# Attention outputs of the first token tile kept on chip, their stores moved to another queue, and five weight splits moved

## The reference

```python
def _attn_ref(q, k, v):                       # q, k, v: 8 x 8 heads x 576 x 64, float32
    scores = scale * np.matmul(q, k.transpose(0, 1, 3, 2))
    Dmat = np.where(rel >= 0, gamma[:, None, None] ** rel[None, :, :], 0.0)
    return np.matmul(scores * Dmat[None, :, :, :], v)
def _moe_ref(x, w1, w2, w3, w_out):           # x: 4608 x 512, d_ff 768
    h = np.maximum(np.maximum(x @ w1, x @ w2), x @ w3)
    return h @ w_out
def _moe2_ref(x, w1, w2, w3, w_out):          # d_ff 1024
    a = x @ w1
    b = x @ w2
    h = a * b @ w3
    return h @ w_out
```

## Time and profile before

| | us |
|---|---|
| median of 3 runs | 1257.79 |
| lowest, highest run | 1256.33, 1263.64 |
| profiled execution | 1263.11 |
| its span, first to last instruction | 1261.3 |
| first matmul of stage B starts at | 193.04 |

### The profile page before, as it was taken

How to read it: one execution, slowest core, us unless ns; L and a number is a source line. 1 busy time by engine, 2 the same in 40 slices (tenths; PEclk the granted TensorE clock), 3 DMA queues, 4 the chain that set the end, 5 groups by cost and what they waited for, 6 DMA issues and landing times. The chain is left out here.

```text
span 1261.3 us, 21125 instructions
## 1 busy us (share of the span) xinstructions
PE 1229.0 (97%) x8288; PEld 1211.0 (96%) x8288; DVE 774.1 (61%) x1186; ACT 487.2 (39%) x771; POOL 434.0 (34%) x228
## 2 busy tenths in 40 slices
PE   7899999999999999999999999999999999999999
PEld 7798889999999999999999999999999999999998
DVE  5565676764645454558789767554545465867563
ACT  3333344432323242426455444242424243545441
POOL 2635536502020202033786564202020216266540
PEclk9899999999999999999999999999999999999999
DMA  9899865212020302033545441212121343444441
GB/s 328 313 333 349 297 235 160 86 47 79 26 101 26 100 26 95 32 126 126 192 163 198 163 169 57 102 64 106 50 101 57 107 156 123 151 150 151 156 157 64
DMA packets 87828, 174.15 MB, mean 138 GB/s; under 512 B 9648, under 2 KB 58416, under 8 KB 87728
## 3 DMA queue, kind: packets, MB, share of 16 engines
q1 hardware_dynamic: 79088, 163.94, 37.0%
q10 hardware_dynamic: 8640, 8.85, 2.0%
HBM read 109.32 MB, written 63.44 MB: 137 GB/s over the span
## 5 line engine op out<-in xcount | busy, mean ns | idle before, releaser
L1057 PE MATMUL ps<-chi,whi 128*128 128x384 f32 x2016 | 675.5, 335 | 11.6 <-DVE clo L795 5.9
L1059 PE MATMUL ps<-chi,wlo 128*128 128x384 f32 x2016 | 674.1, 334 | 0.0
L1058 PE MATMUL ps<-clo,whi 128*128 128x384 f32 x2016 | 674.1, 334 | 0.0
L554 POOL TENSOR_TENSOR raw<-raw,raw 128x768 f32<-128x768 f32 (+2 forms) x96 | 267.3, 2804 | 591.5 <-DMA raw<-xd 222.1
L1057 PEld LDWEIGHTS ps<-chi,whi 128*128 128x128 f32 x2016 | 378.9, 188 | 15.8 <-issue 7.9
L1058 PEld LDWEIGHTS ps<-clo,whi 128*128 128x128 f32 x2016 | 378.9, 188 | 0.0
L1059 PEld LDWEIGHTS ps<-chi,wlo 128*128 128x128 f32 x2016 | 378.9, 188 | 0.0
L795 DVE TENSOR_TENSOR clo<-raw,chi 128x768 fp32r<-128x768 f32 (+2 forms) x168 | 251.9, 1527 | 27.7 <-ACT chi L712 27.7
L712 ACT CAST chi<-raw 128x768 fp32r<-128x768 f32 (+2 forms) x168 | 180.3, 1080 | 86.0 <-PE ps L1059 52.3
L785 ACT COPY w<-ps 128x384 f32<-128x384 f32 x126 | 60.7, 482 | 253.4 <-PE ps L1059 252.0
L771 ACT COPY u<-ps 128x384 f32<-128x384 f32 x126 | 60.8, 482 | 161.8 <-PE ps L1059 160.1
(11 more groups left out here) (41 smaller groups left out, 857.0 us busy)
## 6 DMA issues: line engine op xcount, KB each, us to landing
qks<-qk SPq DMA_DIRECT2D x32, 576.0 KB, 7.0
gd<-h SPq DMA_DIRECT2D x96, 192.0 KB, 1.9
raw<-gd SPq DMA_DIRECT2D x24, 768.0 KB, 5.9
hd<-h SPq DMA_DIRECT2D x72, 192.0 KB, 1.9
raw<-hd SPq DMA_DIRECT2D x24, 576.0 KB, 5.6
vs<-vv SPq DMA_DIRECT2D x32, 320.0 KB, 8.4
raw<-xd SPq DMA_DIRECT2D x24, 384.0 KB, 5.7
x2d<-h SPq DMA_DIRECT2D x48, 192.0 KB, 2.1
```

Of the source, the lines that this page charges most:

```text
L554: return nc.gpsimd.tensor_tensor(out_, a, b, op)
L1057: nc.tensor.matmul(to, w1, x1, start=(start and k == 0), stop=False, skip_group_check=True)
L1058: nc.tensor.matmul(to, w1, x2, start=False, stop=False, skip_group_check=True)
L1059: last = nc.tensor.matmul(to, w2, x1, start=False, stop=(k == KH[st] - 1), skip_group_check=True)
```

## The change

1. **The first tile stays on chip.** `TILE0` lists, for batches 0 and 1, which columns of a pair belong to tile 0. `read_values` copies them from PSUM into the blocks `raw[B]` themselves, in place of `xst`. Pairs 0 to 3 are wholly in tile 0 (two copies, of 384 and 192 columns, no store). Of pairs 4 to 7, 192 columns are (one copy there, one of 384 columns into `xst`, one store). `load_raw(0)` is gone; what waited for it waits for the copies.
2. **Stores from SP, three buffers.** `xst` has three buffers and all 52 stores are issued by SP, in the step's order behind the `vs` load of the same turn. `ks` moves behind u3, uo and the weights.
3. **Values without zero rows.** `vs` is loaded as 128 rows of 512 (`vv`) and 64 rows of 128 (`vt`); DVE zeroes the rest once (six memsets).
4. **Splits moved.** Weights 9, 10, 19 and 20 are split one iteration earlier, 11, 12 and 13 at another place (both halves at the end of `it` where they were in `it` and `it`+1); weight 20 is loaded one iteration earlier; three entries of stage O's table of token splits are moved (`HI_IO`, `LO_IO`).

```diff
-HI_IO = {("prev", "w"): [0], ("end", "u"): [1], ("end", "p3"): [2], ("end", "p2"): [3],
+HI_IO = {("prev", "p3"): [0], ("end", "u"): [1], ("end", "p3"): [2], ("end", "p2"): [3],
...
-LO_IO = {("end", "21"): [0], ("end", "12"): [1], ("next", "22"): [2, 3], ("next", "12"): [4, 5, 6]}
+LO_IO = {("prev", "12"): [0], ("end", "12"): [1], ("next", "22"): [2, 3], ("next", "21"): [4],
+         ("next", "12"): [5, 6]}
...
-             18: 69, 19: 109, 20: 112}
+             18: 69, 19: 109, 20: 111}
...
-W_SPLIT_AT = {wi: it + (wi >= FIRST_W[C]) for wi, it in W_SUM_AT.items()}
+W_SPLIT_AT = {wi: it + (FIRST_W[I] <= wi < FIRST_W[O]) for wi, it in W_SUM_AT.items()}
+
+AT_ONCE = (11, 12, 13)
...
-P1_RAW = 9
+
+TILE0 = [[(0, N, {0: 0, 1: 2}, 0), (N, SEQ, {0: 3, 1: 6}, 0)], [(0, 2 * N - SEQ, {0: 3, 1: 6}, SEQ - N)]]
+X_STORES = [0 if n < PAIRS else 1 if n < 2 * PAIRS else 2 for n in range(NP)]
...
-        xst = at("xst", [P, 2, SEQ], f32, H_AT)
+        xst = at("xst", [P, 3, SEQ], f32, A21_AT + 3 * KH[B] * P * 4)
...
-                sp.dma_start(vs[n % 6][:, :], vv[n, :, :]).then_inc(v_loaded[n % 6], 16)
+                sp.dma_start(vs[n % 6][:, 0:NC * CH], vv[n, :, :]).then_inc(v_loaded[n % 6], 16)
+                sp.dma_start(vs[n % 6][TAIL:P, NC * CH:], vt[n, :, :]).then_inc(v_loaded[n % 6], 16)
...
             for m in range(STEPS):
-                for n in made_in(m + 1):
-                    load_k(n)
                 if m in U3_LOAD:
                     load_u3(U3_LOAD[m])
...
                 if m in P1_W_LOAD:
                     load_weight(P1_W_LOAD[m])
-                if m == P1_RAW:
-                    load_raw(0)
+                for n in made_in(m + 1):
+                    load_k(n)
                 for n in made_in(m + 2):
                     load_qk(n)
                 for n in (2 * m, 2 * m + 1):
                     if n + 4 < NP:
                         load_v(n + 4)
+                    if n - 2 >= PAIRS:
+                        store_x(n - 2)
...
             def read_values(n):
+                b, p = divmod(n, PAIRS)
                 act.wait_ge(valued, n + 1)
-                if n >= 2:
-                    act.wait_ge(x_stored[n % 2], 32 * (n // 2))
-                nc.scalar.copy(xst[:, n % 2, :],
-                               ps[:, 2 * (n % 2):2 * (n % 2) + 2, :].rearrange("p a b -> p (a b)")[:, 0:SEQ]
-                               ).then_inc(x_out, 1)
...
+                x = ps[:, 2 * (n % 2):2 * (n % 2) + 2, :].rearrange("p a b -> p (a b)")
+                in_tile = TILE0[b] if b < 2 else []
+                for i, (lo, hi, block, to) in enumerate(in_tile):
+                    copy = nc.scalar.copy(raw[B][block[p // 2]][:, p % 2, to:to + hi - lo], x[:, lo:hi])
+                if X_STORES[n]:
+                    if n - 3 >= PAIRS:
+                        act.wait_ge(x_stored[n % 3], 16 * x_stores(n - 3))
+                    lo = in_tile[-1][1] if in_tile else 0
+                    copy = nc.scalar.copy(xst[:, n % 3, lo:SEQ], x[:, lo:SEQ])
+                copy.then_inc(x_out, 1)
...
                 for wi in range(2, NW):
-                    if W_SPLIT_AT.get(wi) == it - 1:
+                    if W_SPLIT_AT.get(wi) == it - 1 and wi not in AT_ONCE:
                         split_weight(wi, 0)
...
+                for wi in AT_ONCE:
+                    if W_SPLIT_AT[wi] == it:
+                        split_weight(wi, 0)
+                        split_weight(wi, 1)
```

More of the change, by code:

```diff
@@ L189, with x_stores @@
 P1_W_LO = {12: (0, 0), 13: (0, 1), 14: (1, 0), 15: (1, 1)}
-P1_RAW = 9
+TILE0 = [[(0, N, {0: 0, 1: 2}, 0), (N, SEQ, {0: 3, 1: 6}, 0)], [(0, 2 * N - SEQ, {0: 3, 1: 6}, SEQ - N)]]
+X_STORES = [0 if n < PAIRS else 1 if n < 2 * PAIRS else 2 for n in range(NP)]
+def x_stores(n):
+    return sum(X_STORES[i] for i in range(n % 3, n + 1, 3))
 P1_T = {10: 0, 11: 1, 12: 2, 13: 3}
@@ L309, in build @@
         x_out = sem("x_out")
-        x_stored = [sem(f"x_stored{i}") for i in range(2)]
+        x_stored = [sem(f"x_stored{i}") for i in range(3)]
         uo_loaded = [sem(f"uo_loaded{i}") for i in range(4)]
@@ L378, in store_x @@
                 cut = N if b % 2 == 0 else SEQ - N
-                for i, (lo, hi) in enumerate(((0, cut), (cut, SEQ))):
-                    to = 0 if (b % 2 == 0 or i == 1) else N - cut
-                    sp.dma_start(acts[B][half + i, p // 2, :, p % 2, to:to + hi - lo], xst[:, n % 2, lo:hi]
-                                 ).then_inc(x_stored[n % 2], 16)
+                pieces = ((0, cut, 0 if b % 2 == 0 else N - cut), (cut, SEQ, 0))
+                for i, (lo, hi, to) in enumerate(pieces):
+                    if i >= 2 - X_STORES[n]:
+                        sp.dma_start(acts[B][half + i, p // 2, :, p % 2, to:to + hi - lo], xst[:, n % 3, lo:hi]
+                                     ).then_inc(x_stored[n % 3], 16)
             def load_u3(kb):
@@ L431, in load_raw @@
                 if st == B:
-                    for i in range(2):
-                        sp.wait_ge(x_stored[i], 32 * (4 if t == 0 else NP // 2))
+                    for n in range(NP - 3, NP):
+                        sp.wait_ge(x_stored[n % 3], 16 * x_stores(n))
                 else:
@@ L760, in _ @@
                     else:
-                        for i in range(2):
-                            act.wait_ge(x_stored[i], 32 * NP // 2)
+                        for n in range(NP - 3, NP):
+                            act.wait_ge(x_stored[n % 3], 16 * x_stores(n))
                     nc.scalar.copy(H[1][0][:, :], ps[:, X[g % 2], 0:N]).then_inc(copied21, 1)
@@ L786, in _ @@
                 for wi in range(2, NW):
-                    if W_SPLIT_AT.get(wi) == it:
+                    if W_SPLIT_AT.get(wi) == it and wi not in AT_ONCE:
                         split_weight(wi, 0)
@@ L849, in _ @@
                 nc.vector.memset(state[i][:, :, :], 0.0).then_inc(zeroed, 1)
-            dve.wait_ge(zeroed, 6)
+            for i in range(6):
+                nc.vector.memset(vs[i][0:TAIL, NC * CH:], 0.0).then_inc(zeroed, 1)
+            dve.wait_ge(zeroed, 12)
             for m in range(STEPS):
@@ L932, in _ @@
                         else:
-                            for i in range(2):
-                                dve.wait_ge(x_stored[i], 32 * NP // 2)
+                            for n in range(NP - 3, NP):
+                                dve.wait_ge(x_stored[n % 3], 16 * x_stores(n))
                     nc.vector.tensor_tensor(to[:, :], ps[:, Y[it % 2], 0:N], sbuf_s[it % 2][:, :], ALU.add
@@ L1116 @@
     v2, k2 = by_pair(v), by_pair(k)
-    gap = np.zeros((NP, CH - TAIL, P), np.float32)
     def blocks(w, n, units):
@@ L1127 @@
         "qk": np.concatenate([rows(q), rows(k)], axis=2),
-        "vv": np.concatenate([chunks(v2[:, :NC * CH]), chunks(np.concatenate([gap, v2[:, NC * CH:]], axis=1))], axis=2),
+        "vv": chunks(v2[:, :NC * CH]),
+        "vt": v2[:, NC * CH:],
         "kk": chunks(k2[:, :NC * CH]),
```

36 lines of the change are left out of this document (13 added, 23 removed).

## The result

| | before | after |
|---|---|---|
| median, us | 1258.14 (4 runs, 1256.33 to 1263.64) | 1246.56 (4 runs, 1245.86 to 1247.18) |
| profiled execution | 1263.11 | 1245.86 |
| its span | 1261.3 | 1244.1 |
| first matmul of stage B at | 193.04 | 178.88 |
| from there to the end of the span | 1068.3 | 1065.2 |

The ratio is 0.990, with a 95% interval of 0.987 to 0.993: 11.6 us faster, about 1%, and the interval leaves out no change. The forecast was 1241.5 us, with a range of 1233 to 1250. Between the two profiled executions the attention gave 14.2 us (15.0 were worked out) and the stages behind it 3.1 us (3.8 were worked out).

The account below looks back on a forecast made before the run. PE, busy 97% of the span, was taken as the bound. 15.0 us in the attention and 3.8 us behind it came off 1263.1 us, giving 1244.3; half the profile's 5.3 us excess off gave 1241.5 us, range 1233 to 1250.

Parts of the forecast that it names:

- Store waits and buffers, -7.0 and -4.1 us: Attention: PE's waits on ACT's copies, held up by stores, save 7.0 us; step 3's slow matmuls save 4.1 us.
- stores late: Rival, chance 0.14: stores or loads late on the shared queue, half the attention's gain stays, 7.5 us less, 1249 us.
- Load of tile 0, -2.75 and -1.7 us: Attention, step 11: without this load, the 2.75 us gap waiting for `qks` and 1.7 us of slower matmuls go.
- 0.5 us left for `qks` and `ks`: Attention, early steps: `qks` of step 3 and `ks` of step 2 land close to their need; 0.5 us of loss allowed.
- Load on the queue: Attention, steady steps: 3.28 MB moved per step of 10.12 us, 3% less than before; no cost counted.
- slower: Rival, chance 0.04: one queue moves under 324 GB/s and all 13 full steps grow; 1267 us at 270 GB/s.
- Weight 9, +4.8 us: Before P3 of unit 51: the moved split waits for POOL's combine; new gap 3.2 us, slow matmuls 1.6 us.
- Weight 10, -1.9 us: Behind the attention: split one iteration earlier in DVE's idle time; 2.4 us go, a later token split costs about 0.5.
- Weights 11 to 13, -4.6 us: Low splits moved away from POOL's combine: 6.6 us of gaps and slow matmuls go, 2.0 us left.
- Weights 19, 20 and stage O's table, -2.1 us: Stage O's first three iterations lose 4.5 us of excess; `wlo19` in POOL's combine costs 2.4 us at unit 111.
- The offset, -2.65 us: Half of the 5.3 us by which the profiled execution exceeded the median, taken off 1244.3 us to reach 1241.5 us.
- the splits collide more: Rival, chance 0.17: weights 11 to 13 lose 2.5 us each; behind the attention 5 us worse, 1250 us.

Follow-up runs that it names:

- two half-kernels: The changed kernel with all split tables as before, 1249.2 us, and the kernel before with the moved splits alone, 1256.79 us.
- tile0_only: The kernel before with only tile 0's outputs copied on chip, without their stores and load; two buffers, stores from ACT, old tables: 1252.85 us, ratio 0.9935.
- zeros_back: The changed kernel with values loaded in one DMA again, zero rows included, without DVE's six memsets: 1246.01 us.
- splits_only: The kernel before with the moved splits alone, the attention as before: 1256.79 us, ratio 0.997.
- act_zeros: The kernel of zeros_back with stores issued by ACT behind its two copies of the step, still three buffers: 1244.81 us, ratio 0.988 to before.
- second profile of before: The kernel before, unchanged, profiled a second time: 1258.47 us, stage B starting at 186.30 us.
- w9_w19_back: The changed kernel with weights 9 and 19 split one iteration later, as before: 1244.91 us, ratio 0.987 to before.
- i_half: The changed kernel with the second halves of the splits of weights 11 to 13 one iteration later: 1246.42 us.
- pool_halves: The changed kernel with each combine operation of POOL issued as two, over 192 columns each: 1246.45 us, ratio 0.990 to before.

## Why the prediction was right, and where it was not

1. *Bound and place.* Right. PE was the bound, the attention's stalls were what could go, and the two half-kernels show that the parts add up.
2. *Store waits and buffers, -7.0 and -4.1 us.* Nearly right. Step 3 is whole. But the wait did not vanish: 1.4 us are left in steps 14 and 15, since a store leaves SP 5.5 to 6.3 us after its copy. The landing time was put at 4 to 8 us and is 5.3; the time until the issue was left out. It is the rival "stores late" at a fifth of its size. The "0.9 MB less" in front of step 3's `qks` is 0.79 MB by its own terms (576 KB and six times 32 KB), 2.1 us and not 2.4; the load was in time all the same.
3. *Load of tile 0, -2.75 and -1.7 us.* Right: step 11 starts without a gap at full clock. By medians, `tile0_only` shows that most of the attention's gain hangs on tile 0, with its stores and its load, and not on the queue or the third buffer.
4. *0.5 us left for `qks` and `ks`.* The size was right, the place wrong. Both loads that were thought close landed in time. 0.7 us were lost at 9 us instead, where one more DMA is issued ahead of the second `qks` (`zeros_back`). The count of issues was made for a steady step, where it fits, and not for the start.
5. *Load on the queue.* Right: the steps from 3 to 12 take 10.12 to 10.22 us and step 13 takes 10.37, so the rival "slower" did not come.
6. *Weight 9, +4.8 us.* Right mechanism, 3.96 us measured: gap 2.16 where 3.2 was worked out, and 1.8 of slow matmuls where 1.6 was. The turns came in the order worked out and were 1.0 us shorter in all. That the slow matmuls came is in part luck: at this place they also came behind gaps of 2.07 to 2.16 us in three other profiles, but not behind 2.37 us in `splits_only` (excess 2.66) nor behind 2.06 us in `act_zeros` (excess 2.33).
7. *Weight 10, -1.9 us.* 1.26 us. Iteration 55 held 2.45 us and now holds none, as worked out. But what "a later token split costs back" was put at 0.5 us and is 1.2: iteration 54 held 0.15 us and now holds 1.34, in three small gaps, of which the longest, 0.37 us, waits for `clo`.
8. *Weights 11 to 13, -4.6 us.* 3.25 us. The iterations held 6.57 us and still hold 3.32, where 2.0 was left. The step that failed is "later ones should start a little ahead of POOL": they do, but each second half still waits for a whole combine operation, in all three, and PE's gap behind L897 is 0.7 to 0.9 us each time.
9. *Weights 19, 20 and stage O's table, -2.1 us.* 2.7 us: the 4.5 us of iterations 114 to 116 are gone, and the 1.8 us of iteration 112 are new, with a gap of 1.51 where 2.1 was worked out, and hardly any slow matmuls behind it. The four terms make -3.96 + 1.26 + 3.25 + 2.7 = 3.2 us, against 3.1 between the two profiles.
10. *The offset, -2.65 us.* This was the largest miss, over half of the 5.1 us between the forecast and the measured median. The sum on the profile's own basis, 1244.3 us, is 1.6 us from the profiled 1245.86. Then half of the 5.3 us by which the profiled execution lay above the median was taken off, though the excess sat in the attention's stalls, which the sum had already taken away in full. Taking it off again counted it twice. The second profile of before starts stage B 6.7 us earlier, 5.8 us of it in these stalls, and behind the attention the first was even the quicker one by 2.1 us: as far as two profiles can tell, that is where the excess sat. The right use of it was the other way: a gain of 18.8 us from a bad execution is smaller from the median, and the forecast stays 1244.3.

The chances stood too far to the side of "faster by over 1%" for the same reason: without the offset the forecast would have lain 0.9 us from that bound, and the measured median is 1.0 us past it (0.99 x 1258.14 = 1245.6), with an interval that reaches over it to both sides. So the forecast was in its range, but the likelier side of that bound was the wrong one. The rival "the splits collide more" has a price that its words don't give: if weights 11 to 13 lose 7.5 us where 4.6 were to be gained, it is 1253.6 us, and if they still hold 7.5 us where 2.0 was left, it is 1247.0, not 1250. It did not come.

On the mechanism of items 6 to 9, the Trainium skill (SBUF — State Buffer, Who interferes with whom) has an exclusive lock held for a whole instruction. By that rule, the runs agree: halving POOL's instructions took DVE's merge from 2.40 to 1.43 us.

## What to carry to other kernels

A gain worked out from one execution belongs to that execution: if its excess over the median lies in the very stalls that a change removes, leave the forecast on the profile's basis and take nothing off again. Where two engines wait for each other's whole instructions, moving an instruction mostly moves the wait: five moves together gained 3.3 us, two further tries (`w9_w19_back`, `i_half`) nothing. A shorter instruction on the engine that has time to spare removed it at two places, and on the engine that had none it cost as much (`pool_halves`). When stores change queue, ask first what stands in front of the issue, and only then how long the transfer takes.

## What was not expected of the hardware

A gap of about 2 us may or may not be followed by a stretch at a lower granted clock, and the same program shows both. Behind the 2.16 us above, PE's matmuls take 0.52 us; behind 2.06 us at the same place in `act_zeros`:

```profile
560.70 0.44 PE L1086 MATMUL ps<-chi,whi 128*128 128x384 f32 x1 [2.06 <-DVE h L908]
560.98 0.34 PE L1087 MATMUL ps<-clo,whi 128*128 128x384 f32 x1
```

The windows behind the two gaps (stretch, length, PE busy, granted clock, DMA share, GB/s), first of the changed kernel, then of `act_zeros`:

```profile
565.00:570.00 5.00, 5.00 (x24) 0.75 0.00 0
```

```profile
561.00:566.00 5.00, 5.00 (x30) 1.00 0.02 8
```

The first stretch spent a part at the 1.2 GHz level, the second stayed at 2.4 GHz throughout. It is worth about 1.6 us a time: iteration 4 has a gap of 1.79 us and 2.07 us of excess in the first profile of before, 1.88 and 3.74 us in the second. The gap's length alone does not decide it: 3.20 us before unit 112 in `w9_w19_back` have 0.3 us of slow matmuls behind them, 1.78 us before unit 62 in `zeros_back` have 2.3 us. What does is open, and a single profile's excess behind such a gap is uncertain by that much.
